# Counts of the last two token tiles summed by TensorE, and the ranks of the expert choice kept in PSUM

## The chip, the cores and the metric

The kernel runs on one core of one Trainium2 chip. The metric is the device time of one execution in microseconds (us), lower is better. The engines are named as the profile names them: PE is TensorE (PEld its weight loads), DVE is VectorE, ACT is ScalarE, POOL is GpSimd, SP is SyncE, which here only issues DMAs.

## The reference

Three stages run one after the other on 1536 tokens (2 batches of 768) with 512 features:

```
# 1 attention with a decaying state, 8 heads of 64
state = gamma * state + outer(k[t], v[t]);  y[t] = scale * q[t] @ state
# 2 mixture of 8 experts, one expert a token, capacity 384 rows an expert
logits = x @ w_gate;  expert = argmax(logits)
pos = number of earlier tokens with the same expert;  keep = pos < capacity
h = relu(disp @ w1);  y = h @ w2;  out = gate * y[expert, pos]   (0 if not kept)
# 3 feed-forward with a rational function
h = x @ w_in;  g = P(h) / (Q(h) + 1e-6);  return g @ w_out
```

The change is in stage 2, in `argmax` (the first of equal logits wins) and in `pos`.

## The kernel before, in words

**Tiles.** The tokens are worked in NT = 12 tiles of 128, one token a partition. Stage 1 and the routing of stage 2 are one pipeline over the tiles, written out in order for each engine: `pe_tile`, `act_tile`, `dve_tile` do step t of attention and the routing of tile t - 1. The last three tiles (9, 10, 11; `LAST = 3`) have an order of their own: `pe_last_tiles` and `dve_last_tiles`. Then come the 8 experts (`experts`, from L1071), two row tiles (`NMAIN = 2`) an expert, and the 64 blocks of stage 3. Each engine runs its own list in order; they are tied by semaphores alone. There is no scheduler and no table of costs.

**Routing of a tile.** For tile t, with E = 8 experts:

- PE sums the logits of the tile into columns 0 to 7 of a PSUM bank (`pe_logits_sum`, L373): bank 7 (in `up_high`) for tiles 0 to 10, bank 0 (in `up_low`) for tile 11.
- DVE chooses (`dve_choose`, L510 to L521): copy of the logits to SBUF, their maximum, `rankv` = (logit is the maximum) * (8 - expert), its maximum, and `hot_all[:, t, :]` = the one-hot choice in bf16. For the last three tiles also `mine`, whether the token goes to expert 0.
- PE makes positions (`pe_positions`, L395 and L396): a strictly triangular matrix of ones times `hot_all` of this tile (the earlier tokens of the tile), plus ones times `cum` (all earlier tiles), into columns 8 to 15 of bank 7. It waits for the choice of the tile and for the counts of all earlier tiles.
- DVE picks the token's own position (`dve_place`, L529), adds the tile to the counts (`dve_count`, L534: `cum += hot_all[:, t]`, in bf16), and makes `lane_hot` and `tok` (`dve_lane`, `dve_put`, L540 to L555), from which PE makes the table of row numbers (`pe_index`, L408).

**Last tiles and first expert.** The rows of expert 0 that lie in tiles 0 to 8 are gathered from DRAM (`pool_x_stored`, L906, to `xd`), and PE transposes them (`pe_x_stored`, L417). Those of tiles 9 to 11 are picked on chip: DVE makes a selecting matrix (`dve_fit`, L565) from position and `mine`, and PE multiplies the tile's rows with it (`pe_x_late`, L432 and L434), in a high and a low half. ACT writes `xt` and its rounded high half `xtH` (L472, L474), POOL the low half `xtL` = `xt` - `xtH` (`pool_low_rows`, L896). ACT and DVE then split the sum into `xHL` (L941, L947), and PE begins expert 0 (`pe_up_first`, L1002 and L1010). Between its two halves stands `pe_counts`: the last `pe_index` and the crowding test's sum (L725, ones times `cum`), whose maximum (`dve_crowd`, L819) decides whether an expert has over 256 rows and a second pass is needed. The gathers of expert 1 on (L888) wait for `index`, which DVE copies out (L578) after all the `tok`.

**Queues.** SP loads q, k, v, stores the x rows (L1747) and loads weights (L854, L862); before the store of tile 11 it waits for the gathered rows of expert 0 (L1774).

The orders around the change are these:

```
dve_last_tiles:  ... choose(10) logits_apart(11) place(10) fit(1) count(10)
                 choose(11) place(11) fit(2) count(11) lane(10) put(10) lane(11) put(11) ...
pe_last_tiles:   ... x_late(0, first half) positions(10) logits_sum(11) x_late(0, second half)
                 index(9) x_late(1) positions(11) x_stored x_late(2) index(10)
```

Of the kernel before, what the change touches and what calls it, by code (L numbers as in the profile page):

```python
# [10 lines left out]
ALU = mybir.AluOpType  # L11
ACT = mybir.ActivationFunctionType
AX = mybir.AxisListType
# [15 lines left out]
def build_program(nc, q, k, v, w_gate, w1, w2, w_in, w_out, coef_a, coef_b, consts, out, capacity):  # L29
# [36 lines left out]
    with ExitStack() as ctx:  # L66
# [23 lines left out]
        pt_all = sb(ctx, "pt_all", [P, NT])  # L90
        off_all = sb(ctx, "off_all", [P, NT])
        over_all = sb(ctx, "over_all", [P, NT])
        rankv = sb(ctx, "rankv", [P, E])
        rmax = sb(ctx, "rmax", [P, 1])
        cum = sb(ctx, "cum", [P, E], BF16)
        junk = sb(ctx, "junk", [P, E])
# [282 lines left out]
        def pe_rows(t):  # L379
# [7 lines left out]
                last = e.transpose(rows_place(t, kk), xT[t % 2][:, kk, :], ident)  # L387
            last.then_inc(s_xp, 1)

        def pe_positions(t):  # L390
            e = nc.tensor
            e.wait_ge(s_hot, t + 1)
            wait(e, s_cum, t)
            e.wait_ge(s_lc, t + 1)
            e.matmul(bank[7][:, E:2 * E], before[:, :], hot_all[:, t, :], start=True, stop=False)  # L395
            e.matmul(bank[7][:, E:2 * E], ones[:, :], cum[:, :], start=False, stop=True).then_inc(s_ps, 1)  # L396

        def pe_index(t):
# [106 lines left out]
        def dve_choose(t):  # L505

            e = nc.vector
            e.wait_ge(s_lg, t + 1)
            logits = gate_bank(t)[:, 0:E]
            e.tensor_copy(lg_all[:, t, :], logits).then_inc(s_lc, 1)  # L510
            e.wait_ge(s_lc, t + 1)
            e.tensor_reduce(mx_all[:, t:t + 1], lg_all[:, t, :], AX.X, ALU.max).then_inc(s_pick, 1)
            e.wait_ge(s_pick, 3 * t + 1)
            e.scalar_tensor_tensor(out=rankv[:, :], in0=logits, scalar=mx_all[:, t:t + 1], in1=cc("rank"),
                                   op0=ALU.is_equal, op1=ALU.mult).then_inc(s_pick, 1)
            e.wait_ge(s_pick, 3 * t + 2)
            e.tensor_reduce(rmax[:, :], rankv[:, :], AX.X, ALU.max).then_inc(s_pick, 1)
            e.wait_ge(s_pick, 3 * t + 3)
            e.tensor_scalar(hot_all[:, t, :], rankv[:, :], rmax[:, :], None, ALU.is_equal).then_inc(s_hot, 1)
            if t >= NT - LAST:  # L520
                e.tensor_scalar(mine[t - (NT - LAST)][:, :], rankv[:, 0:1], rmax[:, :], None, ALU.is_equal).then_inc(s_fit, 1)  # L521

        def dve_place(t):

# [194 lines left out]
        def pe_counts():  # L719

            e = nc.tensor
            pe_index(NT - 1)
            e.wait_ge(s_cum, NT)
            e.wait_ge(s_pc, NT)
            e.matmul(bank[7][:, 2 * E:3 * E], ones[:, :], cum[:, :], start=True, stop=True).then_inc(s_cnt, 1)  # L725

        SPLIT_FROM = 3

# [55 lines left out]
        def dve_last_tiles():  # L784
            late = NT - LAST
            dve_logits_apart(late)
            dve_choose(late)
            for c in range(late - SPLIT_FROM, 2 * WC - 1):
                dve_first_half(c)
            dve_index0()  # L790
            dve_mask(NT - 1)
            dve_place(late)
            dve_fit(0)
            dve_count(late)
            dve_lane(late)
            dve_put(late)
            dve_logits_apart(late + 1)
            dve_choose(late + 1)
            dve_logits_apart(late + 2)
            dve_place(late + 1)  # L800
            dve_fit(1)
            dve_count(late + 1)
            dve_choose(late + 2)
            dve_place(late + 2)
            dve_fit(2)
            dve_count(late + 2)
            dve_lane(late + 1)
            dve_put(late + 1)
            dve_lane(late + 2)
            dve_put(late + 2)  # L810
            dve_xL_first()
            dve_index()
            dve_crowd()
            dve_first_half(2 * WC - 1)
# [1186 lines left out]
```

## Time and profile before

| what | value |
|---|---|
| median of 3 runs | 537.9 us (537.85 to 539.23) |
| profiled execution, its own time | 535.94 us |
| its span | 534.1 us |
| PE, DVE, ACT, POOL busy, share of the span | 98%, 80%, 62%, 14% |
| instructions | 8720 |

The span runs from the first to the last instruction of the core. The time of the execution is 1.8 us more, and is the number to set beside the runs. Busy shares are averages over all stages; what one wait costs is read from the stretch in which it stands. All times of the trace are us from the start of the span.

### The profile page before, as it was taken

What the parts mean: (1) busy time and instruction counts of PE and PEld (TensorE: products, weight loads), DVE (VectorE), ACT (ScalarE), POOL (GpSimd) and SP (SyncE); (2) the same over time, 40 slices, a digit from 0 to 9 for tenths busy, and PEclk for the clock granted to TensorE, in tenths of its full rate; (3) what the DMA queues carried; (4) which work ended last, traced back from release to release, by engine and by line L of the source; (5) the groups of instructions that cost most, each with busy time, mean ns of one, the idle gap of its engine ahead of it and who ended that gap; (6) DMA issues with size and microseconds to landing.
All of it is one profiled execution on the core that took longest, in us unless ns stands there. A gap on an engine that the chain in (4) does not pass through costs nothing.

```text
span 534.1 us, 8720 instructions
## 1 busy us (share of the span) xinstructions
PE 524.5 (98%) x3201; PEld 437.7 (82%) x3201; DVE 424.8 (80%) x759; ACT 329.4 (62%) x508; POOL 76.6 (14%) x74
## 2 busy tenths in 40 slices
PE   7999999999999999999999999999999999999997
PEld 5888878888888888888788888888888888888885
DVE  3678788694866759477989999998888888787886
ACT  2454546574655747558869867657576566655652
POOL 2433343350101101003010010004000000200000
PEclk9999999999999999999999999999999999999999
DMA  9999959959959495903060000003000000200002
GB/s 193 227 267 247 293 197 393 395 144 391 380 220 316 143 326 148 398 24 101 23 217 1 1 23 17 1 1 116 4 21 20 1 0 1 80 0 1 0 1 79
DMA packets 65055, 72.26 MB, mean 135 GB/s; under 512 B 41202, under 2 KB 41714, under 8 KB 65012
## 3 DMA queue, kind: packets, MB, share of 16 engines
q1 hardware_dynamic: 58596, 57.96, 34.8%
q0 software_dynamic: 3136, 9.46, 5.2%
q10 hardware_dynamic: 3280, 4.28, 2.3%
q8 instruction: 25, 0.41, 0.3%
q14 instruction: 18, 0.15, 0.1%
HBM read 59.09 MB, written 12.60 MB: 134 GB/s over the span
## 4 chain that ended last, share of the span: by engine, by line
PE 92%; SPq 2%; DMA 2%; DVE 1%; issue 1%; ACT 0%; POOL 0%; ACTq 0%
PE up_low L952 8%; PE up_low L954 7%; PE up_low L953 7%; PE bank L954 6%; PE bank L953 6%; PE bank L952 6%; PE up_high L958 6%; PE up_low L958 5%; PE yrows L952 4%; PE up_high L954 4%; PE yrows L954 4%; PE yrows L953 4%; PE up_high L952 4%; PE up_high L953 4%; PE up_high L959 3%; PE up_low L959 3%
## 5 line engine op out<-in xcount | busy, mean ns | idle before, releaser
L879 DVE TENSOR_TENSOR T<-raw,T 128x1024 fp32r<-128x1024 f32 x60 | 71.5, 1222 | 33.8 <-ACT T L873 33.8
L873 ACT ACTIVATE T<-raw 128x1024 fp32r<-128x1024 f32 x60 | 60.5, 1069 | 32.2 <-PE bank L954 31.8
L952 PE MATMUL up_low<-x2H,T 128*128 128x512 f32 x176 | 69.3, 394 | 0.0
L954 PE MATMUL up_low<-x2H,T 128*128 128x512 f32 x176 | 68.6, 390 | 0.0
L953 PE MATMUL up_low<-x2L,T 128*128 128x512 f32 x176 | 68.5, 389 | 0.0
L1532 ACT ACTIVATE sq<-up_low 128x512 f32<-128x512 f32 x44 | 26.2, 596 | 64.5 <-PE up_low L954 64.3
L1553 DVE SCALAR_TENSOR_TENSOR wa<-sq,coef,wa 128x512 f32<-128x512 f32 x48 | 36.2, 754 | 28.8 <-ACT wa L1534 28.8
L952 PE MATMUL bank<-T,hL 128*128 128x512 f32 x128 | 50.6, 395 | 0.0
L954 PE MATMUL bank<-T,hH 128*128 128x512 f32 x128 | 49.9, 390 | 0.0
L953 PE MATMUL bank<-T,hH 128*128 128x512 f32 x128 | 49.8, 389 | 0.0
L1546 ACT ACTIVATE rc<-wa,cst 128x512 f32<-128x512 f32 x48 | 34.8, 725 | 20.6 <-DVE wa L1553 15.7
L958 PE MATMUL up_high<-xHL,T 128*128 128x512 f32 x128 | 45.8, 398 | 0.0
L958 PE MATMUL up_low<-xHL,T 128*128 128x512 f32 x120 | 42.9, 398 | 0.0
L954 PEld LDWEIGHTS up_low<-x2H,T 128*128 128x128 f32 x176 | 33.0, 188 | 7.0
L952 PEld LDWEIGHTS up_low<-x2H,T 128*128 128x128 f32 x176 | 33.0, 188 | 6.8 <-issue 0.2
L953 PEld LDWEIGHTS up_low<-x2L,T 128*128 128x128 f32 x176 | 33.1, 188 | 6.7
L952 PE MATMUL yrows<-T,gL 128*128 128x512 f32 x96 | 37.5, 391 | 0.0
L954 PE MATMUL up_high<-T,gH 128*128 128x512 f32 x96 | 37.4, 390 | 0.0
L954 PE MATMUL yrows<-T,gH 128*128 128x512 f32 x96 | 37.4, 389 | 0.0
L953 PE MATMUL yrows<-T,gH 128*128 128x512 f32 x96 | 37.4, 389 | 0.0
L952 PE MATMUL up_high<-T,gL 128*128 128x512 f32 x96 | 37.4, 389 | 0.0
L953 PE MATMUL up_high<-T,gH 128*128 128x512 f32 x96 | 37.3, 389 | 0.0
(205 smaller groups left out, 1230.2 us busy)
## 6 DMA issues: line engine op xcount, KB each, us to landing
raw<-in_moe_w_dram SPq DMA_DIRECT2D x14, 2048.0 KB, 10.9
raw<-in_moe_w_dram SPq DMA_DIRECT2D x8, 512.0 KB, 5.1
w_out_raw<-in_moe_w_out_dram SPq DMA_DIRECT2D x4, 1024.0 KB, 16.9
ybuf<-ysb ACTq DMA_DIRECT2D x15, 256.0 KB, 5.6
qin<-in_q_dram SPq DMA_DIRECT2D x12, 256.0 KB, 5.2
kin<-in_k_dram SPq DMA_DIRECT2D x12, 256.0 KB, 5.8
vin<-in_v_dram SPq DMA_DIRECT2D x12, 256.0 KB, 5.8
xbuf<-xt SPq DMA_DIRECT2D x12, 256.0 KB, 4.1
```

The costliest lines, as they stand in the source:

```text
L873: e.activation(W[w][:, 0, cols], raws[par][:, w, cols], ACT.Copy).then_inc(r.wH[w], 1)
L879: e.tensor_tensor(W[w][:, 1, cols], raws[par][:, w, cols], W[w][:, 0, cols].bitcast(F32), ALU.subtract).then_inc(r.wL[w], 1)
L952: nc.tensor.matmul(out_, aL, bH, start=start, stop=False)
L953: nc.tensor.matmul(out_, aH, bL, start=False, stop=False)
L954: return nc.tensor.matmul(out_, aH, bH, start=False, stop=stop)
L958: nc.tensor.matmul(out_[:, 0:2 * n], aH, b, start=start, stop=False)
L959: return nc.tensor.matmul(out_[:, n:2 * n], aL, b[:, 0, :], start=False, stop=stop)
L1532: e.activation(sq[o][:, :], h[:, :], ACT.Square).then_inc(s_w, 1)
L1546: e.activation(rc[o][:, :], wa[o][:, :], ACT.Ln, bias=cc("qeps")).then_inc(s_rc, 1)
L1553: e.scalar_tensor_tensor(out=wa[n % 2][:, :], in0=sq[n % 2][:, :], scalar=coef[:, 5:6], in1=wa[n % 2][:, :], op0=ALU.mult, op1=ALU.add).th ...
```

## The change

Tiles 10 and 11 are no longer added to `cum` by DVE. `cum` stops at ten tiles (`COUNTED = NT - 2`); the positions sum of tile 11 adds ones times `hot_all` of tile 10 as a matmul of its own, and the crowding test's sum adds those of tiles 10 and 11. The ranks go to columns 24 to 31 of the tile's PSUM bank instead of to the SBUF tile `rankv`. `mine` is copied from column 0 of `hot_all`, behind a wait for it, instead of being worked out from the ranks a second time.

```
-        rankv = sb(ctx, "rankv", [P, E])
...
+        COUNTED = NT - 2
+
         def pe_positions(t):
             e = nc.tensor
             e.wait_ge(s_hot, t + 1)
-            wait(e, s_cum, t)
+            wait(e, s_cum, min(t, COUNTED))
             e.wait_ge(s_lc, t + 1)
             e.matmul(bank[7][:, E:2 * E], before[:, :], hot_all[:, t, :], start=True, stop=False)
+            for u in range(COUNTED, t):
+                e.matmul(bank[7][:, E:2 * E], ones[:, :], hot_all[:, u, :], start=False, stop=False)
             e.matmul(bank[7][:, E:2 * E], ones[:, :], cum[:, :], start=False, stop=True).then_inc(s_ps, 1)
...
-            logits = gate_bank(t)[:, 0:E]
+            logits, rankv = gate_bank(t)[:, 0:E], gate_bank(t)[:, 3 * E:4 * E]
...
-            e.scalar_tensor_tensor(out=rankv[:, :], in0=logits, scalar=mx_all[:, t:t + 1], in1=cc("rank"),
+            e.scalar_tensor_tensor(out=rankv, in0=logits, scalar=mx_all[:, t:t + 1], in1=cc("rank"),
                                    op0=ALU.is_equal, op1=ALU.mult).then_inc(s_pick, 1)
             e.wait_ge(s_pick, 3 * t + 2)
-            e.tensor_reduce(rmax[:, :], rankv[:, :], AX.X, ALU.max).then_inc(s_pick, 1)
+            e.tensor_reduce(rmax[:, :], rankv, AX.X, ALU.max).then_inc(s_pick, 1)
             e.wait_ge(s_pick, 3 * t + 3)
-            e.tensor_scalar(hot_all[:, t, :], rankv[:, :], rmax[:, :], None, ALU.is_equal).then_inc(s_hot, 1)
+            e.tensor_scalar(hot_all[:, t, :], rankv, rmax[:, :], None, ALU.is_equal).then_inc(s_hot, 1)
             if t >= NT - LAST:
-                e.tensor_scalar(mine[t - (NT - LAST)][:, :], rankv[:, 0:1], rmax[:, :], None, ALU.is_equal).then_inc(s_fit, 1)
+                e.wait_ge(s_hot, t + 1)
+                e.tensor_copy(mine[t - (NT - LAST)][:, :], hot_all[:, t, 0:1]).then_inc(s_fit, 1)
...
             pe_index(NT - 1)
-            e.wait_ge(s_cum, NT)
+            e.wait_ge(s_cum, COUNTED)
             e.wait_ge(s_pc, NT)
-            e.matmul(bank[7][:, 2 * E:3 * E], ones[:, :], cum[:, :], start=True, stop=True).then_inc(s_cnt, 1)
+            for u in range(COUNTED, NT):
+                e.matmul(bank[7][:, 2 * E:3 * E], ones[:, :], hot_all[:, u, :], start=u == COUNTED, stop=False)
+            e.matmul(bank[7][:, 2 * E:3 * E], ones[:, :], cum[:, :], start=False, stop=True).then_inc(s_cnt, 1)
...
             dve_fit(1)
-            dve_count(late + 1)
             dve_choose(late + 2)
             dve_place(late + 2)
             dve_fit(2)
-            dve_count(late + 2)
```

On VectorE, from the fit of tile 10 to the fit of tile 11, the order before is this:

```order
182 L565 TENSOR_SCALAR fit<-slot_no,pt_all,mine 128x256
183 L534 TENSOR_TENSOR cum<-cum,hot_all 128x8
184 L510 COPY lg_all<-up_low 128x8
185 L512 TENSOR_REDUCE mx_all<-lg_all 128x1
186 L514 SCALAR_TENSOR_TENSOR rankv<-up_low,mx_all,cst 128x8
187 L517 TENSOR_REDUCE rmax<-rankv 128x1
188 L519 TENSOR_SCALAR hot_all<-rankv,rmax 128x8
189 L521 TENSOR_SCALAR mine<-rankv,rmax 128x1
190 L529 SCALAR_TENSOR_TENSOR junk,pt_all<-up_high,hot_all 128x8
191 L565 TENSOR_SCALAR fit<-slot_no,pt_all,mine 128x256
```

In the changed kernel the same stretch reads so (its lines are numbered up to 4 higher):

```order
182 L569 TENSOR_SCALAR fit<-slot_no,pt_all,mine 128x256
183 L513 COPY lg_all<-up_low 128x8
184 L515 TENSOR_REDUCE mx_all<-lg_all 128x1
185 L517 SCALAR_TENSOR_TENSOR up_low<-up_low,mx_all,cst 128x8
186 L520 TENSOR_REDUCE rmax<-up_low 128x1
187 L522 TENSOR_SCALAR hot_all<-up_low,rmax 128x8
188 L525 CAST mine<-hot_all 128x1
189 L533 SCALAR_TENSOR_TENSOR junk,pt_all<-up_high,hot_all 128x8
190 L569 TENSOR_SCALAR fit<-slot_no,pt_all,mine 128x256
```

The count between the fit and the choice is gone, and the rank step, its maximum and the one-hot step work on the PSUM tile `up_low`.

On PE, from the late rows of tile 10 to the transposes of the gathered rows, the changed kernel has:

```order
154 L437 MATMUL bank<-fit,xtH 128x256
155 L396 MATMUL up_high<-hot_all,before 128x8
156 L398 MATMUL up_high<-hot_all,ones 128x8
157 L399 MATMUL up_high<-cum,ones 128x8
158 L420 MATMUL bank<-cst,xd 128x128 x8
```

The middle one of the three sums is new (L398); the two beside it are L395 and L396 of before.

## Rows read from the trace of the kernel before

**Rows 1.** The page, busy time of PE: us, share, instructions.
```profile
PE 524.5 (98%) x3201; PEld 437.7 (82%) x3201; DVE 424.8 (80%) x759; ACT 329.4 (62%) x508; POOL 76.6 (14%) x74
```
**Rows 2.** Chain of waits, last tiles to expert 0: start us, us, what.
```profile
73.66 0.71 DVE fit L565
74.37 1.16 DVE cum L534
...
76.58 0.18 PE up_high L395
...
78.30 0.61 ACT xHL L941
...
79.04 1.19 PE up_low L1002 x8
```
**Rows 3.** Waits of PE, 58 to 92 us: us in total, times, longest.
```profile
PE up_high L395 <- DVE hot_all L519: 0.9, 1, 0.9
```
**Rows 4.** Lines L534 and L565 alone: min/median/max ns, first and last start.
```profile
L534 DVE TENSOR_TENSOR cum<-cum,hot_all x12: 155/159/1237, 18.5 to 77.4; 128x8 bf16<-128x8 bf16 x12
L565 DVE TENSOR_SCALAR fit<-slot_no,pt_all,mine x3: 411/414/711, 69.6 to 77.0; 128x256 fp32r<-128x256 f32 x3
```
**Rows 5.** Timeline of POOL, the two subtractions: first alone, then both merged.
```profile
72.94 1.28 POOL L896 TENSOR_TENSOR xtL<-xt,xtH 128x512 fp32r<-128x512 f32 x1 [1.09 <-ACT xtH L474]
...
72.94 2.57 POOL L896 TENSOR_TENSOR xtL<-xt,xtH 128x512 fp32r<-128x512 f32 x2 [1.09 <-ACT xtH L474]
```
**Rows 6.** Timeline of POOL and DVE, choice of tile 0.
```profile
16.41 1.04 POOL L642 TENSOR_TENSOR qs<-qin,cst 128x512 f32<-128x512 f32 x1
...
16.49 0.17 DVE L510 COPY lg_all<-up_high 128x8 f32<-128x8 f32 x1 [0.48 <-PE up_high L373]
...
17.15 0.16 DVE L517 TENSOR_REDUCE rmax<-rankv 128x1 f32<-128x8 f32 x1
```
**Rows 7.** Timeline of DVE, choice of tile 10 and end of tile 11's.
```profile
72.37 0.23 DVE L514 SCALAR_TENSOR_TENSOR rankv<-up_high,mx_all,cst 128x8 f32<-128x8 f32 x1
72.64 0.16 DVE L517 TENSOR_REDUCE rmax<-rankv 128x1 f32<-128x8 f32 x1
72.83 0.23 DVE L519 TENSOR_SCALAR hot_all<-rankv,rmax 128x8 bf16<-128x8 f32 x1
72.97 0.21 DVE L521 TENSOR_SCALAR mine<-rankv,rmax 128x1 f32<-128x1 f32 x1
73.09 0.28 DVE L503 COPY lgT<-up_low 128x128 f32<-128x128 f32 x1
...
76.29 0.23 DVE L519 TENSOR_SCALAR hot_all<-rankv,rmax 128x8 bf16<-128x8 f32 x1
```
**Rows 8.** Timeline of PE around the late rows of tile 10.
```profile
73.43 0.39 PE L373 MATMUL up_low<-pick,lgT 128*128 128x8 f32 x2
...
74.47 0.36 PE L432 MATMUL bank<-fit,xtL 128*128 128x256 f32 x1
...
75.38 0.28 PE L434 MATMUL bank<-fit,xtH 128*128 128x256 f32 x1
...
76.64 1.07 PE L417 MATMUL bank<-cst,xd 128*128 128x128 f32 x8
```
**Rows 9.** Timeline of SP's queue, the store of tile 11.
```profile
75.01 0.32 SPq L1747 DMA_DIRECT2D xbuf<-xt  x1
```
**Rows 10.** Line L819 alone, a reduce of PSUM.
```profile
L819 DVE TENSOR_REDUCE crowd<-up_high x1: 155/155/155, 80.6 to 80.6; 128x1 int32<-128x8 f32 x1
```
**Rows 11.** Waits of PE's weight loads, 80 us to the end.
```profile
PEld yrows L1315 <- ACT wa L1311: 0.5, 2, 0.3
...
PEld yrows L916 <- DMA xd<-xbuf,index: 0.3, 1, 0.3
```
**Rows 12.** Line L888, 81 to 84 us; then busy time by engine, 80 to 90 us.
```profile
DMA to landing us min/median/max: 6.9/7.3/7.8
...
80.00:90.00 10.00, 10.00 (x58) 8.60 (x58) 8.55 (x13) 6.32 (x10) 2.75 (x2) 1.00 1.02 386
```

## The prediction

> **What bounds the kernel now.** I read the engine totals first: TensorE (PE) is busy for 98% of the span [rows 1], so a change pays only where it closes a gap of PE or shortens what PE itself runs. Next the chain of waits that ended last. It lies on PE nearly everywhere, and leaves it once in this part of the program: VectorE's fit for tile 10, then the count of tile 10, then the choice of tile 11, then back to PE's positions sum for tile 11 [rows 2]. The table of waits confirms a gap: PE stood 0.9 us before that sum, waiting for the choice (`hot_all`, L519) [rows 3]. The question is why a count of eight bf16 numbers takes 1.24 us when eleven other counts take about 0.16 us [rows 4]. The timeline of GpSimd answers it. Two subtractions for the low halves of the x rows (L896) run back to back, 72.94 to 74.22 and from there to 75.51 [rows 5]. The count ends at 75.53 [rows 2], with the second subtraction. The fit before it, 0.71 us where its sister takes 0.41, ends 0.15 us after the first one does [rows 2, 4]. So an instruction of VectorE that takes two inputs from SBUF, or moves SBUF to SBUF, is held while GpSimd works.
>
> Which ones are held matters, because in the changed kernel the choice of tile 11 falls under the same subtraction. Tile 0 shows it: GpSimd worked from 16.41 to 17.45, and under it the first four steps of a choice (copy of the logits 0.17, reduce, rank, reduce 0.16) ran at their usual lengths [rows 6]. Each has at most one tensor input in SBUF. The SBUF page of the Trainium skill (State Buffer, "Who interferes with whom") says the same of two-input instructions, and adds that a copy or `tensor_scalar` from SBUF to SBUF can take both ports. By that rule the last step, if its ranks were in SBUF, would be held until 75.51; from PSUM it runs free. No row shows a `tensor_scalar` from PSUM beside GpSimd's work; I take it as free, like the four steps that the rows show, and price the other case below.
>
> **The change, part by part.** All times are those of the profiled execution.
>
> *Counts of tiles 10 and 11 removed.* The chain gives the count 1.16 us of its own [rows 2]. Without it the choice of tile 11 starts after the fit, and ends not at 76.29 + 0.23 = 76.52 but at 75.36 [rows 7]. PE starts 0.06 after the choice (76.58 against 76.52), so it could start at 75.42.
>
> *What PE can use of it.* Ahead of the positions sum PE does tile 10's eight products of the late x rows. The last starts at 75.38, one every 0.12 us, so PE is free at 75.50 [rows 8]. PE, not VectorE, is then the later one, by 0.08. The gain there is 76.58 - 75.50 = 1.08 us, which is a ceiling. The eight transposes behind the sum need gathered rows; SP's store, which waits for their landing, was issued at 75.01 [rows 9], so they don't bind. The late products of tile 11 need the second subtraction (75.51) and a fit that hangs on the positions sum and moves with it. From there the chain is PE, ScalarE's `xHL` (L941), PE again, all relative to one another [rows 2].
>
> *Matmuls added.* One in the positions sum of tile 11, two in the crowding test: three. Between the first of the two matmuls at 76.58 and what follows at 76.64 lie 0.06 us [rows 2, 8], so 0.03 each, 0.09 in all, paid on PE. Bounds: nothing, and 0.18 each if none overlapped, 0.54. I take 0.09, since these follow the same kind of matmul with weights loaded beside them.
>
> *Ranks written to and read from PSUM.* A reduce of eight PSUM columns took 0.155 (L819), of eight SBUF columns 0.16 [rows 7, 10]: nothing. The rank step reads PSUM and writes SBUF in 0.23; the last step takes 0.23 from SBUF [rows 7]. The nearest rows from PSUM are 0.155 for a reduce and 0.28 for a copy of 128 columns [rows 7, 10], so the last step costs between -0.08 and +0.05, the rank write the same; I take zero for both. Up to 0.08 of delay is free, since PE is later by that.
>
> VectorE's cost page (VectorE: DVE Perf Modes, the section on the TRN2 errata) gives a fixed 58 cycles from SBUF and 120 from PSUM at 0.96 GHz. By that the two reads cost 0.13 us more, the choice ends at 75.49, PE starts at 75.55, and the sum would be 0.94 instead of 0.99. The reduce row above speaks against it.
>
> *`mine` made by a copy behind a wait.* Today it starts before the choice's last step has ended (72.97 against 73.06) and is followed 0.12 later by the copy of tile 11's logits (73.09). A dependent step starts 0.03 after its source's end (72.80 to 72.83) [rows 7], so `mine` now starts at 73.09. Its own issue distance is the 0.12 of today or, for a shorter form, less. The copy behind it is thus up to 0.12 late, and PE's sum of tile 11's logits, at 73.43 directly behind it [rows 8], with it. That is covered: PE next stands for the fit of tile 10 (end 74.37, PE 74.47), and that fit is held by the first subtraction to 74.22 however much later than 73.66 it arrives. For tile 9 the delay meets the mask of tile 11; PE shows no wait for a mask, so nothing, at most 0.1. For tile 11, `mine` starts at 75.39 and may be held to 75.51; VectorE's next work waits for PE's sum anyway, which starts at 75.50. If that cover failed the cost is 0.1.
>
> *Counts earlier in time.* The positions sum waits for ten counts instead of eleven; those of tiles 0 to 9 stay. VectorE's lane work starts earlier still, by the second removed count (0.16 or less), and feeds nothing that PE waits for.
>
> *Sum.* 1.08 - 0.09 = 0.99, say **1.0 us**, bounds 0.3 to 1.1.
>
> *Does it survive to the end?* After 80 us PE shows only small waits, and they are of compute on compute, apart from 0.3 us for the first expert loop's gathered rows [rows 11]. Those rows were landed 6.9 and 7.8 us after issue, while the 16 DMA engines were full from 80 to 90 us [rows 12]. The gather hangs on `index`, which moves by the same 1.0, and the queues are full in both places, so I let it land 1.0 earlier. The granted clock is at full speed in that stretch (1.00), which is the 2.4 GHz level, and PE idles less than before.
>
> The profiled execution took 535.94 us (span 534.1 plus 1.8 around it) and would take 534.9. The median of the three runs, 537.9, lies 1.96 above the profiled one; I keep that distance, so **536.9 us**, 0.19% less. The measurement can tell about 0.3%, or 1.6 us, so the forecast is "no difference that can be told".
>
> **Rivals.**
>
> *The gather is the next thing late.* PE reaches the transposes of expert 1's rows 1.0 us earlier, and already waited 0.3 there [rows 11]. If the landing is set by the full queues and not by the issue, PE waits for it where it stands and all 1.0 is given back: 535.94 and 537.9. For: the queues are full, and landings scatter by 0.9 us. Against: the gather's own distance from issue is bounded work, its issue moves. Chance 0.12.
>
> *Slower: the fit of tile 10 falls behind the second subtraction.* It sits between the two subtractions. Each step of the choice before it that grows delays it. It starts at 73.66; if it came after 74.22 it would be held to 75.51, PE's late products of tile 10 would start at 75.6 instead of 74.47, and the positions sum at 76.65 instead of 76.58. With the added matmuls that is 0.07 + 0.09 = 0.16 slower: 536.1, median 538.1. It decides from a delay of 0.56 us, or of 0.4 if a held instruction must reach the port 0.16 after its start. My delays add to 0.12, and 0.25 with the cost page's PSUM reads. Chance 0.05.
>
> *PSUM is dear.* The cost page's rule as a mechanism here: the last choice ends 0.13 later, 0.05 of it uncovered, gain 0.94: 535.0, median 537.0. Between this and the forecast lies also the case that the step from PSUM is held anyway: the choice ends near 75.53, PE starts at 75.59, gain 0.9. Chance 0.12.
>
> *More than the ceiling, or something the trace of before doesn't show.* A later stall closes too, or the runs scatter: before's three lie between 537.85 and 539.23. Chance 0.07.
>
> **How the numbers follow.** Forecast 0.64, rivals 0.12, 0.05, 0.12, 0.07. The cases lie between 536.9 and 538.1; the scatter of a median of few runs widens that. I give 536.0 to 538.2. Neither the forecast nor any rival reaches 0.3% by itself. Faster by more needs 1.6 us, above the ceiling, so only scatter or the last case: 0.12. Slower by more needs the same from the other side: 0.03. The rest, 0.85, is the same.
>
> **What would show it.** Right: the choice of tile 11 begins near 74.3, its steps keep 0.16 to 0.23 us, PE's wait for that choice goes from 0.9 us to nothing, and the first matmul of expert 0's sums (79.04 now [rows 2]) comes 1.0 earlier; PE's transposes of expert 1's rows too. Wrong: a PE wait for `xd` near 90 us that grew by what was saved (first rival); a fit of tile 10 of over 1 us (second); a choice whose steps grew, or one of them ending at 75.5 (third). If the choice moves by 1.1 and the span doesn't, the gain was given back later and my step on survival is wrong.

## The result: 0.7% faster, and the profile after

| | before | changed |
|---|---|---|
| median of 7 runs each, run in turn | 538.88 us (537.85 to 540.2) | 534.99 us (534.3 to 536.78) |
| profiled execution, own time | 535.94 us | 535.68 us |
| its span | 534.1 us | 533.9 us |
| instructions | 8720 | 8724 |

The ratio is 0.9931, 95% interval 0.9911 to 0.9951: 3.9 us less, about four times the 1.0 us forecast, and the changed kernel's 534.99 us lies below the range given for it. The two profiled executions differ by 0.26 us only, so one of them isn't typical of its kernel, or both. That is a first lesson: what has to be explained is a step from 538.9 to 535.0, and a profile shows one execution only.

The page of the changed kernel, busy time (answers to [rows 1]):

```profile
PE 526.1 (99%) x3204; PEld 439.3 (82%) x3204; DVE 423.8 (79%) x757; ACT 329.0 (62%) x508; POOL 76.3 (14%) x74
```

PE does three matmuls more, VectorE two counts less. What PE waited for, 58 to 92 us (total, times, longest) (answers to [rows 3]):

```profile
PE up_high L372 <- DVE lgT L506: 1.0, 1, 1.0
PE up_low L1006 <- ACT xHL L945: 0.3, 1, 0.3
```

The wait for the choice of tile 11 is gone, as forecast. But a wait of 1.0 us for the copied logits of tile 10 (`lgT`, L506) stands there, which before's trace didn't have. The chain of waits (start, us, what) shows it, and the landmarks of before (answers to [rows 2]):

```profile
68.95 1.61 PE up_high L365 x8
70.55 0.02 issue
70.58 0.30 DVE lgT L506
...
76.05 0.03 PE up_high L396
...
77.97 0.61 ACT xHL L945
...
78.72 1.18 PE up_low L1006 x8
```

Expert 0 begins at 78.72 against 79.04, 0.32 earlier, where I had forecast 1.0. VectorE under the two subtractions of GpSimd (timeline of VectorE, then of GpSimd) (answers to [rows 5, 7]):

```profile
72.48 0.15 DVE L525 CAST mine<-hot_all 128x1 f32<-128x1 bf16 x1
...
73.03 0.54 DVE L569 TENSOR_SCALAR fit<-slot_no,pt_all,mine 128x256 fp32r<-128x256 f32 x1
73.49 0.15 DVE L513 COPY lg_all<-up_low 128x8 f32<-128x8 f32 x1
...
74.35 0.23 DVE L522 TENSOR_SCALAR hot_all<-up_low,rmax 128x8 bf16<-128x8 f32 x1
...
72.14 2.59 POOL L900 TENSOR_TENSOR xtL<-xt,xtH 128x512 fp32r<-128x512 f32 x2 [2.08 <-ACT xtH L477]
```

GpSimd works from 72.14 to 74.73. The whole choice of tile 11, 73.49 to 74.58, lies under it at the usual lengths. The step that I couldn't find a row for, a `tensor_scalar` from PSUM, takes 0.23 and isn't held. Nor is `mine` of tile 10, one column copied from SBUF to SBUF under the first of the two subtractions: 0.15.

So the choice moved as forecast, but this trace does not show where 3.9 us went. Two places differ. The first is the start. What PE waited for in the first 42 us of before:

```profile
PE up_high L669 <- DVE zero L218: 1.5, 1, 1.5
PE up_high L297 <- POOL vs L642: 0.9, 1, 0.9
PE up_low L265 <- DMA kin<-in_k_dram: 0.7, 1, 0.7
PE bank L283 <- ACT qT L458: 0.7, 1, 0.7
PE up_low L265 <- ACT xt L472: 0.6, 1, 0.6
```

and of the changed kernel:

```profile
PE up_high L673 <- DVE zero L217: 1.5, 1, 1.5
PE bank L282 <- ACT qT L461: 0.7, 1, 0.7
PE up_high L296 <- POOL vs L646: 0.2, 1, 0.2
```

Three waits that stem from loads shrink from 2.2 to 0.2 us: two of them (`kin`, `xt`) are gone, and the one for `vs` is down from 0.9 to 0.2. No instruction of that stretch that loads or uses q, k and v was changed. The positions sum of tile 9 starts at 66.11 instead of 67.95. The second place is the clock. Busy time by stretch of the changed kernel (length, then PE, PEld, DVE, ACT, POOL, granted clock, DMA share, GB/s):

```profile
73.00:74.00 1.00, 1.00 (x8) 0.91 (x8) 0.90 (x4) 0.38 (x1) 0.97 (x2) 0.72 0.22 84
74.00:75.00 1.00, 1.00 (x7) 1.00 (x7) 0.66 (x4) 0.00 (x0) 0.73 (x1) 0.50 1.09 301
75.00:76.00 1.00, 1.00 (x9) 0.91 (x8) 0.00 (x0) 0.00 (x0) 0.00 (x0) 0.50 0.90 307
76.00:77.00 1.00, 1.00 (x10) 1.00 (x9) 0.76 (x6) 0.00 (x0) 0.00 (x0) 0.58 0.97 360
```

PE stood for `lgT` until 70.92, and from 73.4 to 76.8 its granted clock is 0.50, the level of 1.2 GHz. So this profile gained 1.8 us by 66 us, and lost 1.0 at `lgT` and more at the low clock. A later profile of the same kernel without the low clock (r9 below) needs 11.2 us from the positions sum of tile 9 to expert 0, this one 12.6: the low clock took 1.4.

### The profile page after: what moved, and what is told of

Its sections match the earlier page's. It is cut to its first block, busy times and chain, and to the rows that moved or that the text cites. A ratio compares the mean times of both kernels' runs of the same rounds, so it can differ in the third digit from the quotient of the medians.

```text
span 533.9 us, 8724 instructions
## 1 busy us (share of the span) xinstructions
PE 526.1 (99%) x3204; PEld 439.3 (82%) x3204; DVE 423.8 (79%) x757; ACT 329.0 (62%) x508; POOL 76.3 (14%) x74
## 4 chain that ended last, share of the span: by engine, by line
PE 96%; DVE 1%; DMA 1%; SPq 1%; issue 0%; POOL 0%; ACT 0%
PE up_low L956 8%; PE up_low L957 8%; PE up_low L958 7%; PE bank L958 6%; PE bank L956 6%; PE bank L957 6%; PE up_high L962 6%; PE up_low L962 5%; PE yrows L956 4%; PE yrows L957 4%; PE up_high L957 4%; PE up_high L958 4%; PE yrows L958 4%; PE up_high L956 4%; PE up_high L963 3%; PE up_low L963 3%
## 5 line engine op out<-in xcount | busy, mean ns | idle before, releaser
L958 PEld LDWEIGHTS up_low<-x2H,T 128*128 128x128 f32 x176 | 33.1, 188 | 7.0
L957 PEld LDWEIGHTS up_low<-x2L,T 128*128 128x128 f32 x176 | 33.1, 188 | 6.6
```

The costliest lines, as they stand in the source:

```text
L957: nc.tensor.matmul(out_, aH, bL, start=False, stop=False)
L958: return nc.tensor.matmul(out_, aH, bH, start=False, stop=stop)
```

## Experiments

There are five sets of runs; each ratio is against the kernel before in the same set on the same chip. A stand, below, is a time in which PE waits. "Held" is said of an instruction of VectorE that lasts until GpSimd's subtraction ends. The theories to tell apart are these. The removed count is worth 1.0 us and PE limits it. Ranks in PSUM are worth nothing, or save a hold. The addresses of the SBUF tiles matter, because the tile `rankv` (32 bytes a partition) is gone and what is allocated behind it lies 32 bytes lower. And PE's stands cost more than their length, through the clock.

### Set 1: each part alone

Before again, unchanged (r1_before_again):

> The kernel before itself, unchanged, to see what its ordinary execution looks like: the profiled execution of before (535.94 us) was faster than all seven timed ones (537.85 to 540.20). Theory A (clock): PE's stand of 0.9 us before tile 11's positions sum is followed, in most executions, by a stretch in which PE is granted less than full clock, costing 2 to 3 us; then a profile at about 538 us shows a granted clock under 1.00 between 70 and 100 us, and its ratio is 1.000. Theory B (start of the program): the executions differ in waits for the first loads, before 40 us, and the clock is 1.00 throughout; then the gain of the change beyond 1.0 us is not from the last tiles.

Measured: 1.0003 (0.9994 to 1.0013), 536.66 us. Before takes 536.91 here, against 538.88 in the runs of the result. The comparison is sound to 0.1%, and the kernel before has a time of its own in each set.

Counts by PE, ranks left in SBUF, all tiles where they were (r2_counts_only):

```
-            wait(e, s_cum, t)
+            wait(e, s_cum, min(t, COUNTED))
...
+            for u in range(COUNTED, t):
+                e.matmul(bank[7][:, E:2 * E], ones[:, :], hot_all[:, u, :], start=False, stop=False)
...
-            dve_count(late + 1)
```

> The counts of tiles 10 and 11 by PE, but the ranks in SBUF and tile membership worked out from them as before. If the gain comes from the removed count and what hangs on it, the ratio is near that of the whole change (0.993), with the choice's last step (SBUF to SBUF) held until GpSimd's second subtraction ends, so that PE starts the positions sum at most 0.1 to 0.2 us later: 0.9932 to 0.9936. If the ranks in PSUM carry the part that I did not forecast, the ratio is 0.997 to 0.999.

Measured: 0.9975 (0.9966 to 0.9984), 1.3 us. The timelines of VectorE, GpSimd and PE:

```profile
75.73 0.41 DVE L523 TENSOR_SCALAR hot_all<-rankv,rmax 128x8 bf16<-128x8 f32 x1
...
73.53 2.58 POOL L900 TENSOR_TENSOR xtL<-xt,xtH 128x512 fp32r<-128x512 f32 x2 [1.08 <-ACT xtH L478]
...
76.20 0.18 PE L397 MATMUL up_high<-hot_all,before 128*128 128x8 bf16 x1
```

The last step of the choice, now SBUF to SBUF under the second subtraction, takes 0.41 instead of 0.23 and ends at 76.14, where GpSimd ended at 76.11. The last late product ahead of PE's sum starts at 75.98, one every 0.12, so PE was free at 76.10 and started at 76.20: ranks in PSUM are worth 0.1 us here. From the positions sum of tile 9 to that of tile 11 it is 7.66 us (68.54 to 76.20), in before 8.63 (67.95 to 76.58): the step is 0.97.

Ranks to PSUM alone, counts as before (r3_ranks_only):

```
-        rankv = sb(ctx, "rankv", [P, E])
...
-            logits = gate_bank(t)[:, 0:E]
+            logits, rankv = gate_bank(t)[:, 0:E], gate_bank(t)[:, 3 * E:4 * E]
```

> The ranks in PSUM and mine copied from the choice, all counts still by VectorE. My theory: the count is still held by the subtraction, nothing gained, ratio 0.9995 to 1.0005. The rival (the ranks in PSUM carry the unforeseen part): ratio 0.994 to 0.996.

Measured: 0.9956 (0.9943 to 0.9969), 2.2 us, from a part that I had priced at nothing. Tile 9 to tile 11 is 8.63 us as in before, the count takes its 1.25, PE waits its 0.9. The positions sum of tile 9 is at 66.51, though: the gain lies wholly ahead of it, where the loads are. In the profiles it is 1.4 us (67.95 to 66.51), since before's profile is 1.0 us faster than its median in this set.

Before with PE kept busy in its gap (r4_before_filled):

```
             pe_x_late(1, range(KD))
+            for _ in range(16):
+                nc.tensor.matmul(bank[1][:, 0:P], ones[:, :], ones[:, :], start=True, stop=True)
             pe_positions(t)
```

> The kernel before, with 16 matmuls of 128x128 bf16 ones (into an unused PSUM bank, read by nobody) ahead of tile 11's positions sum: PE is busy where it stood for 0.9 us, VectorE's held count and all waits stay. Theory A (clock): no lowered clock follows, and most of what the change brought beyond 1.0 us comes without removing the wait, ratio 0.994 to 0.996. Theory B or any theory by which only the earlier choice pays: ratio 1.000 to 1.001.

Measured: 0.9992 (0.9982 to 1.0001). Had the stand of 0.9 us an after-effect of 2 us, filling it would have taken that away. It takes 0 to 1.0 us, so the stand costs little beyond its length. No execution of set 1, with or without the filler, has a mean granted clock under 0.999, so this says nothing of executions that do. So neither the count's stand nor the ranks' own instructions explain the 2.2 us of r3, and the addresses are left.

### Sets 2 and 3: the addresses

I read the addresses from the compiled kernels; no page of the profile shows them. The first buffer of q, k and v starts at 32 modulo 512 bytes in before, and at 0 modulo 512 in the changed kernel. The expert weights (`raw`), `T`, `xt`, `xd` and `ysb` move likewise.

Before with two small tiles sharing one slot, so that all behind lie 32 bytes lower (r5_before_aligned):

```
-        rmax = sb(ctx, "rmax", [P, 1])
...
-        junk2 = sb(ctx, "junk2", [P, ST])
+        pair = sb(ctx, "pair", [P, ST + 1])
+        junk2, rmax = pair[:, 0:ST], pair[:, ST:ST + 1]
```

> The kernel before with one change of SBUF addresses alone: rmax shares the 32-byte slot of junk2, so every tile allocated behind it starts 32 bytes lower, as in the changed kernel (the large tiles start at 0 instead of 32 modulo 512 bytes). Ranks in SBUF, all counts by VectorE. Theory D (addresses): the transfers of q, k, v and x land about 0.7 us sooner, their share of the DMA engines falls from 34.6% to 32.8%, ratio 0.9950 to 0.9962, as with the ranks in PSUM (0.9956). Theory P (the ranks in PSUM themselves make the gain): ratio 0.9990 to 1.0010.

The changed kernel with a pad of 32, 64, 128 or 256 bytes in the place of `rankv` (r6_after_pad32, r7_after_pad64, r11_after_pad128, r8_after_pad256; the pad is 8, 16, 32 or 64 wide):

```
+        sb(ctx, "pad", [P, 8])
```

> The changed kernel with an unused SBUF tile of 32 bytes where rankv was: the addresses of before, everything else changed. Theory D: only the removed counts pay, ratio 0.9970 to 0.9982, that of the counts alone (0.9975). Theory P: ratio 0.993, as the changed kernel.

> The changed kernel with an unused tile of 64 bytes: the large tiles start at 64 modulo 512. If 64 bytes is what a transfer wants, it keeps the changed kernel's ratio, 0.993, and the DMA share of 32.8%. If 512 or 256 bytes, it falls back to 0.9970 to 0.9982 with a share near 34.6%.

> The changed kernel with an unused tile of 128 bytes: the large tiles start at 128 modulo 512. With 64 the gain of the addresses was gone, with 256 it was there. If 128 is enough: ratio as the changed kernel's, share of the DMA engines near 33%; if 256 is wanted: 0.9955 to 0.9980 and near 34.6%.

> The changed kernel with an unused tile of 256 bytes: the large tiles start at 256 modulo 512. If 64 or 256 bytes is what a transfer wants, ratio 0.993 and a share of 32.8%; if 512, 0.9970 to 0.9982 and 34.6%.

The changed kernel again (r9_after_again), and with 32 bytes ahead of the buffers of q, k and v (r12_after_loads_shifted). What stage 1 has behind them in the same block (`qs`, `vs`, `state`, `wg`, `lgT`) moves with them; the weight buffers, `xt` and all else stay:

```
+        sb(att, "pad", [P, 8])
```

> The changed kernel itself, as the mark for the three others of this set: ratio 0.9915 to 0.9945 (0.9931 measured at first).

> The changed kernel with an unused tile of 32 bytes ahead of the q, k and v buffers alone: they start at 32 modulo 512, the weight buffers, the x rows and all else stay at 0. If the gain of the addresses is won by the loads of q, k and v, which PE waits for in the first 40 us: ratio 0.9955 to 0.9980, and the waits for the loads and for GpSimd's vs are back. If the weights' transfers carry it: as the changed kernel, 0.993.

Measured (before: 538.80 in set 2, 538.78 in set 3):

| kernel | start modulo 512 | ratio | interval | share of the DMA engines, loads' queue |
|---|---|---|---|---|
| before, moved | 0 | 0.9961 | 0.9942 to 0.9980 | 33.4% |
| changed, again | 0 | 0.9925 | 0.9896 to 0.9955 | 32.7% |
| changed, pad 256 | 256 | 0.9917 | 0.9891 to 0.9942 | 33.1% |
| changed, pad 32 | 32 | 0.9955 | 0.9938 to 0.9972 | 34.6% |
| changed, pad 64 | 64 | 0.9950 | 0.9925 to 0.9974 | 34.4% |
| changed, pad 128 | 128 | 0.9958 | 0.9941 to 0.9975 | 34.6% |
| changed, stage 1's buffers at 32 | 32, rest 0 | 0.9963 | 0.9944 to 0.9982 | 34.4% |

Moving before's tiles by 32 bytes, with nothing else changed, gives 0.4%; putting them back in the changed kernel takes 0.3 to 0.4% away. A start at 0 or 256 modulo 512 is fast, one at 32, 64 or 128 isn't; and moving stage 1's buffers, which are those of q, k and v in the main, is enough. With starts at 0 or 256 the same bytes occupy the queue for a shorter time.

I had expected 0.9970 to 0.9982 for r6 and r7, the worth of the counts alone in set 1. They came at 0.9955 and 0.9950: in these sets the rest of the change is worth about 2 us, not 1.3. Set 3 and what follows is about that difference.

The clearest sign of the addresses is where the positions sum of tile 9 starts, ahead of all that the edit's instructions change in the last tiles. In the 9 profiles of this document with the buffers at 0 or 256 it starts at 66.11 to 67.24 us, in the 11 others at 67.95 to 69.17; the means lie 1.9 us apart. The DMA view of the first 30 us, queue of the loads (packets, MB, share of 16 engines) and the loads of q, of before:

```profile
q1 hardware_dynamic: 20512, 6.11, 103.3%
...
qin<-in_q_dram SPq DMA_DIRECT2D x7, 256.0 KB, 5.3
```

of the changed kernel:

```profile
q1 hardware_dynamic: 22425, 6.88, 94.8%
...
qin<-in_q_dram SPq DMA_DIRECT2D x8, 256.0 KB, 4.5
```

of the kernel whose stage 1 buffers alone are shifted (r12):

```profile
q1 hardware_dynamic: 20661, 6.15, 104.3%
...
qin<-in_q_dram SPq DMA_DIRECT2D x7, 256.0 KB, 5.4
```

Share times 16 engines times 30 us over packets: 24.2 ns a packet in the first and third, 20.3 in the second. The queue is all but full in the three (94.8% to 104.3%). A packet takes 16% less in the second, and 9% more packets and 13% more bytes were moved in the same 30 us. The Trainium skill (DMA: Bandwidth & Descriptors, How a descriptor splits into AXI transactions) says that when a descriptor does not start on a 256-byte boundary, its first transaction starts at the boundary below; it tells this of reads. Here the side that is out of line is the one written. The rows agree in kind; that the split is the cause was not shown.

There is a second thing in sets 2 and 3. ACT's copy `xT` behind PE and VectorE's copy of tile 10's logits (`lgT`) start late in all eight of their profiles. Two rows of the changed kernel's profile (a set of this kind):

```profile
70.48 0.60 ACT L468 ACTIVATE xT<-up_low 128x512 f32<-128x512 f32 x1 [2.52 <-remote]
...
70.58 0.29 DVE L506 COPY lgT<-up_high 128x128 f32<-128x128 f32 x1 [1.39 <-PE up_high L365]
```

and of the same program in set 5:

```profile
69.75 0.60 ACT L468 ACTIVATE xT<-up_low 128x512 f32<-128x512 f32 x1 [1.02 <-PE up_low L348]
...
70.12 0.29 DVE L506 COPY lgT<-up_high 128x128 f32<-128x128 f32 x1 [0.19 <-PE up_high L365]
```

Counted from the positions sum of tile 9, VectorE's copy starts 1.2 to 1.3 us later and ACT's 1.4 to 1.6 us later than in the profiles without this, behind the same matmuls. I call it the late signal. None of the ten profiles of sets 1, 4 and 5 has it, with the same kernels among them. Before takes 538.8 to 538.9 us in the sets with it (the runs of the result among them) and 536.6 to 536.9 in the others. So the forecast seems to have rested on a profile of before without it and on times with it; that those times had it is inferred from their length.

Counts by PE at the addresses of the changed kernel, ranks left in SBUF (r10_ranks_in_sbuf, set 3; the parts of r2 and r5 together):

> The changed kernel's counts and its SBUF addresses, but the ranks in an SBUF tile (rmax shares the slot of junk2, so nothing behind it moves). The last step of tile 11's choice is then held until GpSimd's second subtraction ends, and PE starts the positions sum 0.1 us later than it is free. Theory D (counts 1.0 to 1.4 us, addresses 2 us, ranks in PSUM next to nothing): ratio within 0.0005 of the changed kernel's, 0.9920 to 0.9950. If the ranks in PSUM have a worth of their own: 0.9955 or more.

Measured: 0.9963 (0.9941 to 0.9986), against 0.9925 for the changed kernel beside it, 2.1 us apart. I had expected the two within 0.0005 of each other, and that is refuted. Timelines of VectorE, GpSimd and PE:

```profile
72.20 1.24 DVE L523 TENSOR_SCALAR hot_all<-rankv,pair 128x8 bf16<-128x8 f32 x1
...
72.14 2.58 POOL L900 TENSOR_TENSOR xtL<-xt,xtH 128x512 fp32r<-128x512 f32 x2 [2.12 <-ACT xtH L478]
...
73.50 0.18 PE L397 MATMUL up_high<-hot_all,before 128*128 128x8 bf16 x1 [0.77 <-DVE hot_all L523]
```

With the late signal the choice of tile 10 ends under the first subtraction. From SBUF its last step is held for 1.24 us and PE stands 0.8 before the positions sum of tile 10; from PSUM it takes 0.23 (72.22 in the changed kernel). The hold also pushes the fit of tile 10 into the second subtraction, to whose end it is held in its turn, and the count behind it comes when both are over. In the moved before (r5), where the subtractions end at 74.68:

```profile
73.90 0.93 DVE L565 TENSOR_SCALAR fit<-slot_no,pt_all,mine 128x256 fp32r<-128x256 f32 x1
74.75 0.15 DVE L534 TENSOR_TENSOR cum<-cum,hot_all 128x8 bf16<-128x8 bf16 x1
```

So with the ranks in SBUF, removing the count gains nothing (r10 0.9963, r5 0.9961), and the 2.1 us come with the ranks in PSUM on top of it.

That does not make them the ranks' alone. No run has the ranks in PSUM, the count kept and the signal late: r14 and r17 below were meant to be that, and fell on the signal on time. The rows of r9 allow an estimate. There the fit of tile 10 is held by the first subtraction alone (73.86 to 74.41), and the second lasts until 75.58. A count kept behind the fit would start near 74.34 and be held to about 75.60, the choice of tile 11 would end at 76.68 instead of 75.42, and PE's sum would start near 76.74 instead of 75.63: 1.1 us later, 9.8 us after that of tile 9, which is r5's distance. By this estimate neither part pays alone when the signal is late, and the two together do.

Of the 2.1 us, 1.2 lie between tile 9 and tile 11 (9.86 us in r5, 8.70 in r9, both at a full clock). Expert 1's gathered rows take up to 0.7 more; the waits of PE beyond 80 us, first r5, then r9:

```profile
PE yrows L916 <- DMA xd<-xbuf,index: 1.2, 1, 1.2
```

```profile
PE yrows L920 <- DMA xd<-xbuf,index: 0.5, 1, 0.5
```

The clock is a third thing, and adds little to that difference: the median of the executions at a mean clock of 0.999 and above is 536.48 us in r10 and 534.46 in r9, still 2.0 apart. Stretches of r10 after its two stands (columns as above):

```profile
73.00:74.00 1.00, 0.40 (x4) 0.30 (x4) 0.96 (x6) 0.38 (x1) 0.96 (x2) 1.00 0.20 74
74.00:75.00 1.00, 1.00 (x6) 0.96 (x5) 0.96 (x3) 0.00 (x0) 0.72 (x1) 0.53 1.19 324
75.00:76.00 1.00, 1.00 (x7) 0.95 (x6) 0.88 (x5) 0.00 (x0) 0.00 (x0) 0.50 0.83 229
76.00:77.00 1.00, 1.00 (x6) 0.91 (x5) 0.00 (x0) 0.00 (x0) 0.00 (x0) 0.50 1.03 393
```

Over the whole core, five of r5's twelve executions and three of r10's had a mean clock of 0.994 (537.4 to 539.7 us, at 0.999 and above 536.3 to 536.7), and 13 of the 52 of before in the two sets (540.4 to 542.5, at 0.999 and above 537.0 to 539.7). None of the 54 executions of the changed kernel and its padded forms in these sets did; three had 0.997. A mean of 0.997 is a low stretch too: the profile of the changed kernel with its 3.4 us at 0.50 has 0.997. Counting all below 0.999, it is 21 of 52 in before, 7 of 12 in r5, 7 of 12 in r10, 3 of the 54, and 2 of the 7 of the result. So the kernels with two stands close together have the low clock in half of the executions or nearly so, those with one stand seldom. For before the low clock explains part of the time: its executions at 0.999 and above have a median of 538.4 and 538.0 us in the two sets, 0.4 and 0.8 under the medians of all.

### Sets 4 and 5: ranks at the old addresses, and a filler

Before a third time (r13_before_third), and ranks in PSUM with a pad in the place of `rankv`, twice (r14, r17):

```
-        rankv = sb(ctx, "rankv", [P, E])
+        sb(ctx, "pad", [P, 8])
```

> The kernel before once more, for its profile. In the profiles since the fifth run PE's signals at tile 10 (the end of tile 11's values and of tile 10's logits) reach ACT and VectorE 1.1 to 1.3 us late, which in the first five profiles they did not, and before takes 538.8 us instead of 536.9. If before has this late signal too, its choice of tile 10 falls under GpSimd's first subtraction, the last step (SBUF to SBUF) is held for 1.2 us, PE stands 0.8 us there, and the count of tile 10 is then NOT held (0.15 us), because both subtractions are over. If the signal is on time, the profile is that of r1: count held 1.24 us, time 536.9.

> The ranks in PSUM, all counts by VectorE, addresses of before (an unused tile of 32 bytes where rankv was). My theory H (two different holds): where the signal is late, the ranks in PSUM free the last step of tile 10's choice, PE does not stand there, the clock stays, and the counts are worth nothing: ratio as r6's, 0.9945 to 0.9970. Where the signal is on time, nothing is gained: 0.9995 to 1.0005. Against it stands the theory that the counts make the gain in both: ratio 0.9990 or more with a late signal.

> As r14, which fell on a chip where the signal was on time and gained nothing (0.9995). If the signal is late here, theory H gives 0.9945 to 0.9970 and no stand of PE before tile 10's positions sum; if it is on time, 0.9990 to 1.0005 again.

The moved before with 14 matmuls ahead of tile 10's positions sum, to fill the stand of r10 there, twice (r15, r18):

```
             pe_x_late(0, range(2))
+            for _ in range(14):
+                nc.tensor.matmul(bank[1][:, 0:P], ones[:, :], ones[:, :], start=True, stop=True)
             pe_positions(t - 1)
```

> The kernel of r5 (before, addresses lowered) with 14 matmuls of ones ahead of tile 10's positions sum, read by nobody, where PE stands 0.8 us for the held choice when the signal is late. Five of r5's twelve executions showed a granted clock of 0.994, and took 537.4 to 539.4 us against 536.4 for those at 1.000. Theory A' (two stands of PE close together lower the clock afterwards): no execution at 0.994, all near 536.4, ratio 0.9945 to 0.9960. If the lowered clock has another cause: as r5, 0.9961, with a third or more of the executions at 0.994.

> As r15, with a late signal: theory A' (two stands of PE close together lower the clock) gives no execution at a granted clock of 0.994, while before in the same set has a quarter of its executions there; otherwise a third or more. With the signal on time: no lowered clock anywhere, ratio 0.996 to 0.998, and the question stays open.

And the changed kernel a third time (r16_after_third):

> The changed kernel once more, as the mark of this set. With a late signal at tile 10 (before at 538.8 us): ratio 0.9915 to 0.9940. With the signal on time (before at 536.7 us) it should be the product of the counts alone (0.9975) and the addresses (0.9956): 0.9920 to 0.9945, and the profile should show tile 11's positions sum 7.55 us after tile 9's (8.63 in before).

Measured, before at 536.59 and 536.84 us:

| kernel | ratio | interval |
|---|---|---|
| r13 before | 1.0002 | 0.9991 to 1.0013 |
| r14 ranks in PSUM, old addresses | 0.9995 | 0.9985 to 1.0006 |
| r17 the same | 0.9999 | 0.9991 to 1.0008 |
| r15 moved before, filled | 0.9971 | 0.9961 to 0.9982 |
| r18 the same | 0.9964 | 0.9953 to 0.9975 |
| r16 changed kernel | 0.9947 | 0.9934 to 0.9960 |

The signal was on time in all six, so the fillers filled nothing and told nothing of the clock. They did something else. Their 14 matmuls pushed the fit of tile 10 into the second subtraction (GpSimd's two together 71.38 to 73.88; r15):

```profile
72.89 1.16 DVE L565 TENSOR_SCALAR fit<-slot_no,pt_all,mine 128x256 fp32r<-128x256 f32 x1
```

It takes 1.16 us instead of 0.41 unheld, and PE waits 0.7 us ahead of tile 10's late products. That is the mechanism of my slower rival, in a kernel that wasn't the one forecast. It also means that r15 and r18 show less than the addresses are worth.

Ranks in PSUM at the old addresses gain nothing, twice. That settles r3: its 2.2 us were the addresses. With the signal on time the changed kernel takes 533.82 us, 3.0 less than before, and its parts are seen alone: counts 1.3 us (r2), addresses 1.4 to 2.2 (r15 and r18 with fillers, r3), ranks 0. The product of r2 and r3 would be 0.9931; r16 measured 0.9947 (0.9934 to 0.9960), a little less than the parts promise. PE's timeline of r16, and all that it waited for in 60 to 80 us:

```profile
74.29 0.28 PE L437 MATMUL bank<-fit,xtH 128*128 128x256 f32 x1
74.41 0.18 PE L396 MATMUL up_high<-hot_all,before 128*128 128x8 bf16 x1
74.45 0.17 PE L398 MATMUL up_high<-hot_all,ones 128*128 128x8 bf16 x1
74.47 0.17 PE L399 MATMUL up_high<-cum,ones 128*128 128x8 bf16 x1
74.50 0.63 PE L420 MATMUL bank<-cst,xd 128*128 128x128 f32 x4
```

```profile
PE up_low L1006 <- ACT xHL L945: 0.3, 1, 0.3
```

The positions sum follows the late products at once, without a stand. Tile 9 to tile 11 is 7.55 us (66.86 to 74.41), 1.08 less than before's, and the earlier start of tile 9's sum adds 1.09 (67.95 to 66.86). No kernel of these runs is faster than the changed one beyond its interval.

A table ties the profiles together: where expert 0 begins (the first matmul on `xHL`), the span, and what is left between them.

| profile | begins | span | rest | PE's wait for `xd` |
|---|---|---|---|---|
| before | 79.04 | 534.1 | 455.1 | 0 |
| r2 | 78.69 | 533.8 | 455.1 | 0 |
| changed | 78.72 | 533.9 | 455.2 | 0 |
| r16 | 76.89 | 532.0 | 455.1 | 0 |
| r3 | 77.60 | 533.1 | 455.5 | 0.2 |
| r9 | 78.12 | 533.8 | 455.7 | 0.5 |
| r10 | 79.62 | 535.7 | 456.1 | 0.7 |
| r5 | 78.44 | 534.7 | 456.3 | 1.2 |

What the change moved lies in the first 79 us, and comes through to the end unless the gathered rows of expert 1 are late.

## Why the prediction was wrong, by its steps

Two terms failed. The first is "I take zero for both", the ranks in PSUM: the edit that moves them also drops `rankv` and so moves the load buffers, which is worth 1.4 to 2.2 us by set, and was put at nothing. The second is the base: the sum was read from a profile with the signal on time, and the median that it was set beside had it late, as far as times can tell. There the count and the ranks together are worth about 2 us (r9 beside r5 and r10, and r6) instead of the 0.99 forecast. The two make up the 3.9 us.

- **Count removed, PE as the limit, 1.08 minus 0.09 for matmuls.** Right in mechanism and size for the execution that was profiled. Forecast 0.99 between tile 9 and tile 11; measured 0.97 (r2) and 1.08 (r16), and 1.3 us (0.9 to 1.8) in time (r2). The three sums start 0.04 and 0.02 apart, near the 0.03 that I took. It holds where the signal is on time. Where it is late and the ranks are in SBUF, the count isn't held and its removal gains nothing (r10 beside r5).
- **Ranks in PSUM, nothing.** The durations were right: over twelve tiles the median rank step went from 226 to 234 ns, its maximum from 161 to 166, the one-hot step from 231 to 226. The Trainium skill (VectorE: DVE Perf Modes, the section on the TRN2 errata) has 62 cycles more from PSUM, by my estimate 65 ns an operation at its 0.96 GHz; the maximum and the one-hot step, which now read PSUM, don't show them. What failed is the step's scope: "I take zero for both" priced the instructions of the edit and not the line that takes the tile `rankv` away. That line moved the load buffers behind it by 32 bytes, and is worth 0.3 to 0.4%, more than the count's 0.25% (r2). And where the signal is late, zero is wrong for the instructions too: from SBUF the last step of tile 10's choice is held 1.24 us, from PSUM it isn't, and r10 and r9 lie 2.1 us apart. No row of before named addresses; but the diff showed the line, and the trace a queue that was full at the start and 2.2 us of PE's waits on loads.
- **The last step held if its ranks were in SBUF.** Right: held 1.24 us in r10, 0.18 too long in r2. The Trainium skill's rule (SBUF — State Buffer, Who interferes with whom) on a `tensor_scalar` from SBUF to SBUF is borne out by these rows. I expected `mine` might be held too; one column under the first subtraction (72.48, 0.15 us) wasn't.
- **`mine` behind a wait, covered.** Right: no wait of PE's came from it.
- **Survival to the end.** Right for the count: r2's span minus the start of expert 0 is before's. The gather rival is a mechanism of this kernel all the same, seen where the program ran ahead or was disturbed (0.2 to 1.2 us), and at 0.3 us in before itself (r13).
- **The base.** "I keep that distance" of 1.96 us between one profile and a median. The distance is more than scatter: before's three runs have the length of the sets with the late signal (538.8 to 538.9 in three sets), its profile has the signal on time. With the signal late the change does another thing: it removes the hold of tile 10's choice, keeps the fit and the count from being held behind it, and goes with fewer executions at the low clock. The forecast's 0.12 for "faster" counted scatter and a closed later stall; what came was a late signal that the trace before didn't show, and the addresses.
- **The rivals.** Gather late: in part, small. Fit behind the second subtraction: not here, but shown by r15. PSUM dear: no. "More than the ceiling, or something the trace of before doesn't show", at 0.07, is what came.

**What stays open.** What makes the signal late in some sets and for tile 10 alone. Sets and not kernels decide it, nor the chip alone: set 1, with the signal on time, and set 3, with it late, ran on the same chip by its number. What ranks in PSUM do with the count kept and the signal late was not run. That before has it in those sets is read from its time and from r5, which has before's instructions; no profile of before itself shows it. Whether the stands cause the low clock: r10 and the changed kernel show one after the other, r5's profile has both stands and a full clock, and the fillers meant to decide came in sets where nothing was late. And why the start of a buffer that is written costs time, at 128 modulo 512 as much as at 32.

## What to carry to other kernels

A diff that adds or drops a small SBUF tile also moves every tile behind it: look at where the large load buffers start, and try them on a 256-byte boundary when the loads' queue is full and PE waits for it. Test such a change with a pad in the dropped tile's place before crediting an instruction. Before pricing a gap, ask whether the timed runs are the execution that the profile shows: a profile that is 2 us faster than all its timed runs doesn't show what they did, and which of two parts pays can depend on it.

## What the runs showed of the hardware

- Loads in pieces of 64 f32 (256 bytes, a head's row) into SBUF buffers: 24.2 ns a packet at a start of 32 modulo 512, 20.3 at 0, with the queue all but full (before and the changed kernel, first 30 us); landing of q 5.3 against 4.5 us. In time of the kernel, starts at 64 and 128 are as slow as 32 (0.9950 and 0.9958 beside 0.9955), and 256 as fast as 0 (0.9917 beside 0.9925).
- A `tensor_scalar` of eight f32 columns from SBUF to SBUF is held by GpSimd's subtraction (1.24 us in r10 instead of 0.23); the same from PSUM isn't (0.23 in the changed kernel), nor is a one-column copy from SBUF to SBUF (0.15).
- Work behind PE started 1.2 to 1.3 us (VectorE) and 1.4 to 1.6 us (ACT) later at one place of the program, in every profile of some sets of runs and in none of others.
- A granted clock of 0.50 (the 1.2 GHz level) for 3.4 us between 73 and 78 us, behind a stand of PE of 1.0 us (the changed kernel), or of 1.0 and 0.8 (r10), in some executions; r5's profile has the same two stands at a full clock. Executions with a mean of 0.994 took 537.4 to 539.7 us in r5 and r10, those at 0.999 and above 536.3 to 536.7.
